# Two cross-attention passes and two MLPs on one core: in each unit of the first MLP the numerator's matmuls move ahead of the next slope's, and GpSimd squares 288 of 960 columns in place of 192

## The chip, the cores and the metric

One core of a Trainium2 chip runs the whole program in one launch. The metric is the device time in microseconds (us); the kernel before takes 2559.63 us (median of 3 runs, 2558.59 to 2561.37). The engines are TensorE (PE in the profile, with its weight loads as PEld), VectorE (DVE), ScalarE (ACT), GpSimd (POOL) and the queue that issues the transfers (SP).

## The reference

`x` is 2 x 12480 tokens of 128 features, `inducing` is 32 x 128. First an attention of the 32 inducing rows over all tokens of a batch (`h = mab(I, x)`), then of all tokens over the 32 rows of `h` (`mab(x, h)`), which gives 24960 x 128 tokens. Two MLPs of width 2048 follow:

```
h = x @ w_in;  h2 = h*h;  h3 = h2*h                     # first MLP
P = a[0] + a[1]*h + a[2]*h2 + a[3]*h3
Q = 1.0 + |b[0]|*|h| + |b[1]|*h2
x = (P / (Q + 1e-6)) @ w_out
h = x @ w_in2;  out = (h * cos(h)) @ w_out2             # second MLP
```

All is float32.

## The kernel before

**Tiling.** Tokens go in 52 groups of 480. A group meets the 2048 hidden features in 8 units; a unit is 2 chunks of 128 features by 480 tokens, that is 128 partitions x 960 columns. So the first MLP has 416 units, and the second as many. Since the token that enters the first MLP is a softmax over 32 rows, `h @ w_in` is folded into small stacked weights (`stack_now`, 96 rows: high part, low part, high part again) that multiply the attention weights (`part_hi`, 96 rows). Three stacks stand there: one gives the hidden value, one the slope (a term linear in h), one the numerator's rest.

**One unit n of the first MLP**, engine by engine:
- TensorE `hidden` (2 matmuls, L1068) writes h into banks 0 and 1, which all units share: it waits until the unit before has been read by `square_ready` and `abs0_ready` (ScalarE) and by `abs1_ready` (VectorE).
- ScalarE `from_hidden`: Square of the first OWN columns of each half (L564; OWN is 384, so 768 of 960 columns), then Abs of the first half (L565, 480 columns). VectorE `absolute` (L790) makes the other 480 columns of |h|; it waits for the Square.
- GpSimd `square_rest` (L409): the other 2 x 96 = 192 columns of the square, from |h|; then `denominator` (L420): square plus |h|, 960 columns.
- ScalarE `log_den` (Ln, L548) and `invert_den` (Exp, L553): one over the denominator.
- TensorE `slope` (2 matmuls) writes into one of two pairs of banks, `num(k)`, taken in turn. It waits for `act_ready` of two units before, that is until the quotient of unit n-2 has been read out of the same banks.
- VectorE `product` (L781) multiplies the slope by the square in place; it waits for `slope_ready` and the square.
- TensorE `numerator` (2 matmuls, L1068 too) adds its stack onto the product; it waits for `prod_ready`.
- VectorE `quotient` (L802) makes the activation; it gives `act_ready`.
- TensorE `end` (2 `matmul` calls that run as 4 passes, L1075) multiplies it by `w_out` into the accumulator; after 8 units ScalarE `keep_y` (L571) reads it out.

**Order.** The order on each engine is written out by hand, one step per k, with units at offsets (HID 5, MAG 4, SLOPE 3, DEN 3, NUM 2, QUO 1). In step k, TensorE does `end(k)`, at most one piece of the next groups' attention (`score2`, L1084, in two steps of 8; `turn_att`, L1092, in two others), `slope(k+3)`, `numerator(k+2)`, `hidden(k+5)`. VectorE does `product(k+2)`, `quotient(k+1)`, `absolute(k+4)`, with small attention operations between (`between`), the largest `keep_att` (L764) behind `absolute`. ScalarE does `log_den(k+2)`, `from_hidden(k+4)`, `invert_den(k+2)`. GpSimd does `square_rest(k+3)`, `denominator(k+3)`, and once per group `part_att` (L425, L427). All are loops over 24 units (3 groups). In 4 of VectorE's rounds (12 groups) it also splits the second MLP's weights (L916, L921) once or twice per group.

The second MLP (L1219 to L1236 and the rest) has its own order and is not touched.

Of the kernel before, what the change touches and what calls it, by code (L numbers as in the profile page):

```python
# [64 lines left out]
TINY_BETA, TINY_SIGMA = 2.0 ** -40, 2.0 ** -46  # L65
SPLIT = GROUP

OWN = 384


HID, MAG, SLOPE, NUM, QUO, DEN = 5, 4, 3, 2, 1, 3
# [18 lines left out]
def group_due(k, at):  # L90
    return (k - at) // GROUP_UNITS if (k - at) % GROUP_UNITS == 0 else None
# [6 lines left out]
def exists_unit(n):  # L98
    return not isinstance(n, int) or 0 <= n < UNITS


def bass_set_attention_two_mlps(nc, x, inducing, w_in, w_out, a, b, w2_in, w2_out, out):
# [3 lines left out]
    with ExitStack() as ctx:  # L106
# [120 lines left out]
        def halves(ap):  # L227
            return ap.rearrange("p (a n) -> p a n", a=2)
# [4 lines left out]
        def num(k):  # L233
            n = 2 + 2 * (k % 2)
            return bank[:, n:n + 2, 0:GROUP]
# [76 lines left out]
        def later(group):  # L312

            return exists(group) and not (isinstance(group, int) and group < 2)
# [78 lines left out]
        def _(pool):  # L393
# [9 lines left out]
            def square_rest(n0, k):  # L403
# [3 lines left out]
                pool.wait_ge(abs1_ready, n + 1)  # L407
                rest = halves(abs_h[k % 3])[:, :, OWN:]
                nc.gpsimd.tensor_tensor(halves(square[k % 3])[:, :, OWN:], rest, rest, ALU.mult).then_inc(square_parted, 1)  # L409

# [100 lines left out]
        def _(act_):  # L511
# [43 lines left out]
            def from_hidden(n0, k):  # L555
# [5 lines left out]
                elif n == 2:  # L561

                    act_.wait_ge(exp_turned, STEPS)
                nc.scalar.activation(halves(square[k % 3])[:, :, 0:OWN], hid[:, :, 0:OWN], ACT.Square).then_inc(square_ready, 1)  # L564
                nc.scalar.activation(abs_h[k % 3][:, 0:SPLIT], bank[:, 0, 0:GROUP], ACT.Abs).then_inc(abs0_ready, 1)  # L565
# [420 lines left out]
        def _(pe):  # L986
# [77 lines left out]
            def from_stack(place_out, i, k, start, stop):  # L1064
                u, place = k % GROUP_UNITS, k // GROUP_UNITS % PLACES
                for t in range(2):
                    w = slice((2 * u + t) * P, (2 * u + t + 1) * P)
                    mm = pe.matmul(place_out[:, t, :], stack_now[:, i, w], part_hi[0:K3, place, :], start=start, stop=stop,  # L1068
                                   skip_group_check=not start)
                return mm  # L1070
# [7 lines left out]
            def score2(g, batch, subs):  # L1078
                if subs[0] == 0:
                    pe.wait_ge(x_fetched, g * 16 + 16)  # L1080
                    if not isinstance(g, int) or g >= 1:
                        pe.wait_ge(att_kept, g)
                for j in subs:
                    mm = pe.matmul(spare[0:SUB, j * M:(j + 1) * M], x_group[:, j * SUB:(j + 1) * SUB], ht[:, batch, :], start=True, stop=True)  # L1084
                if subs[-1] == GROUP_SUBS - 1:
                    mm.then_inc(s2_ready, 1)

            def turn_att(g, subs):
                pe.wait_ge(att_parted, g + 1)
                for j in subs:  # L1090
                    thrice = att[:, j, :, :].rearrange("p r m -> p (r m)")
                    mm = pe.transpose(spare[0:K3, j * SUB:(j + 1) * SUB], thrice, ident[0:SUB, 0:SUB])  # L1092
                if subs[-1] == GROUP_SUBS - 1:
                    mm.then_inc(att_turned, 1)

            def hidden(n0, k):
                n, g = n0 + k, n0 // GROUP_UNITS + k // GROUP_UNITS
                if not isinstance(n, int) or n >= 1:
                    pe.wait_ge(square_ready, n)
                    pe.wait_ge(abs0_ready, n)  # L1100
                    pe.wait_ge(abs1_ready, n)
                else:

                    pe.wait_ge(xt_ready, GROUPS)
                if k % GROUP_UNITS == 0:
                    pe.wait_ge(att_kept, g + 1)
                if isinstance(n, int) and n < GROUP_UNITS:
                    pe.wait_ge(stack_first[PIECES], 2 * PIECES * 16)
                    pe.wait_ge(stack_first[n * 2 * P // PIECE], 16)
                if isinstance(n, int) and 0 <= n - BATCH_GROUPS * GROUP_UNITS < GROUP_UNITS:  # L1110
                    pe.wait_ge(stack_ready[k % GROUP_UNITS], 48)
                from_stack(hid, 0, k, True, True).then_inc(hid_ready, 1)

            def slope(n0, k):
                n = n0 + k
                if not isinstance(n, int) or n >= 2:
                    pe.wait_ge(act_ready, n - 1)
                elif n == 0:

                    pe.wait_ge(exp_ready, STEPS)  # L1120
                else:

                    pe.wait_ge(exp_col_ready, STEPS)
                    pe.wait_ge(h_kept, STEPS)
                from_stack(num(k), 1, k, True, True).then_inc(slope_ready, 1)

            def numerator(n0, k):
                pe.wait_ge(prod_ready, n0 + k + 1)
                from_stack(num(k), 2, k, False, True).then_inc(num_ready, 1)

            def end(n0, k):
                n, g = n0 + k, n0 // GROUP_UNITS + k // GROUP_UNITS
                pe.wait_ge(act_ready, n + 1)
                if k % GROUP_UNITS == 0 and not (isinstance(g, int) and g == 0):
                    pe.wait_ge(y_kept, g)
                product_out(acc, v1, k, act[k % 2]).then_inc(act_used, 1)

            def steps(n0, ks, batch=None):
                for k in ks:
                    if k >= 0:  # L1140
                        end(n0, k)
                    for half in range(2):
                        subs = range(half * GROUP_SUBS // 2, (half + 1) * GROUP_SUBS // 2)
                        g = group_due(k, SCORE + half)
                        if g is not None and later(n0 // GROUP_UNITS + g):
                            group = n0 // GROUP_UNITS + g
                            score2(group, batch if batch is not None else group // BATCH_GROUPS, subs)
                        g = group_due(k, TURN + half)
                        if g is not None and later(n0 // GROUP_UNITS + g):
                            turn_att(n0 // GROUP_UNITS + g, subs)  # L1150
                    if k + SLOPE >= 0 and exists_unit(n0 + (k + SLOPE)):
                        slope(n0, k + SLOPE)
                    if k + NUM >= 0 and exists_unit(n0 + (k + NUM)):
                        numerator(n0, k + NUM)
                    if k + HID >= 0 and exists_unit(n0 + (k + HID)):
                        hidden(n0, k + HID)

# [43 lines left out]
            hidden(0, 3)  # L1201
            fold(1, range(PIECES))
            steps(0, range(-1, 0))
            pe.wait_ge(v1_loaded, 16)
            steps(0, range(0, 1))
            pe.wait_ge(stack_lo, B * STACKS)
            with pe.Fori(0, TURNOVER) as i:
                n0 = pe.snap(i * BODY)
                steps(n0, range(1, BODY + 1), batch=0)
            steps(TURNOVER * BODY, range(1, BODY + 1))  # L1210
            with pe.Fori(TURNOVER + 1, LOOPS) as i:
                n0 = pe.snap(i * BODY)
# [86 lines left out]
            with pe.Fori(0, LOOPS // 2) as i:  # L1299
                n0 = pe.snap(i * 2 * BODY)  # L1300
# [28 lines left out]
```

## Time and profile before

| | |
|---|---|
| median of 3 runs | 2559.63 us |
| the profiled execution's own time | 2556.54 us |
| its span | 2554.7 us |
| TensorE busy / weight loads | 99% / 71% of the span |
| ScalarE | 96% |
| VectorE | 91% |
| GpSimd | 82% |
| granted TensorE clock, mean | 0.999 |
| DMA in the two MLPs | 8 to 17 GB/s in most slices |

Busy time is the time in which at least one operation of the engine is open. Operations of one engine overlap: the next one starts before the end of the one before, so that neither the sum of durations nor a share near 100% tells by itself that an engine has no time left. The first MLP takes about 100 to 1430 us of the span, the second the rest.

### The profile page before, as it was taken

To read this page: it belongs to the slowest core of one execution; us is meant where nothing else is said; L and a number is where in the kernel's file an instruction comes from. 1 tells how busy PE (TensorE), PEld (TensorE's weight loads), DVE (VectorE), ACT (ScalarE), POOL (GpSimd) and SP (SyncE) were. 2 spreads that over 40 slices of the span, in tenths; PEclk is the share of its full clock that TensorE was granted. 3 is DMA by queue.
4 is the path that set the end of the run, shared out by engine and by line. 5 is a ranking of instruction groups with operands and counts; after the bars stand their busy time and mean duration, and the time that the engine had idled before them with its cause. 6 is when DMAs were issued, how large, how long until landed. Compare 5 with 4: busy or idle time off the path is not lost.

```text
span 2554.7 us, 38677 instructions
## 1 busy us (share of the span) xinstructions
PE 2529.0 (99%) x10790; PEld 1812.3 (71%) x10790; DVE 2319.9 (91%) x2712; ACT 2450.9 (96%) x3152; POOL 2101.8 (82%) x1471
## 2 busy tenths in 40 slices
PE   8899999999999999999999999999999999999999
PEld 6566666666666666666665788888888888888887
DVE  5899999999999999999999888888888888888887
ACT  6899999999999999999999999999999999999998
POOL 0588888888888888888888888888888888888886
PEclk9999999999999999999999999999999999999999
DMA  7200000000020000000000000000000000000000
GB/s 223 66 12 8 12 8 12 8 12 8 12 74 16 8 12 8 12 8 12 8 12 1 17 13 12 12 12 12 12 12 12 12 12 12 12 12 12 12 12 16
DMA packets 27816, 48.94 MB, mean 19 GB/s; under 512 B 3352, under 2 KB 12344, under 8 KB 27512
## 3 DMA queue, kind: packets, MB, share of 16 engines
q1 hardware_dynamic: 27768, 48.33, 6.3%
q8 instruction: 26, 0.43, 0.1%
q14 instruction: 22, 0.18, 0.0%
HBM read 18.04 MB, written 12.78 MB: 12 GB/s over the span
## 4 chain that ended last, share of the span: by engine, by line
PE 94%; DVE 3%; issue 2%; DMA 1%; ACT 0%; POOL 0%; SPq 0%; DVEq 0%; POOLq 0%; ACTq 0%
PE bank L1075 24%; PE bank L1068 22%; PE bank L1236 22%; PE bank L1228 21%; PE bank L1084 1%; DVE work L802 1%; PE bank L1219 1%; PE bank L996 1%; PE bank L1092 1%; DMA x_ring<-in_x_dram 1%; PE bank L1025 0%; PE bank L1005 0%; DVE work L790 0%; DVE bank L781 0%; POOL work L420 0%
## 5 line engine op out<-in xcount | busy, mean ns | idle before, releaser
L479 POOL TENSOR_TENSOR act_lo<-work,act_hi 128x960 fp32r<-128x960 f32 (+1 forms) x413 | 831.1, 2013 | 196.7 <-ACT act_hi L647 196.6
L1075 PE MATMUL bank<-work,v 128*128 128x480 f32 x1664 | 737.8, 565 | 0.0
L1068 PE MATMUL bank<-part_hi,stack_now 96*128 96x480 f32 x2496 | 655.4, 397 | 6.5 <-DVE work L802 3.0
L420 POOL TENSOR_TENSOR work<-work 128x960 f32<-128x960 f32 x278 | 621.3, 2235 | 40.7 <-POOL work L409 5.6
L960 DVE SCALAR_TENSOR_TENSOR work<-work,bank 128x960 f32<-128x960 int32 x416 | 479.2, 1152 | 141.5 <-ACT work L634 141.4
L1068 PEld LDWEIGHTS bank<-part_hi,stack_now 96*128 96x128 f32 x2496 | 437.1, 188 | 220.2 <-DVE work L802 167.1
L781 DVE SCALAR_TENSOR_TENSOR bank<-bank,over_c,work 128x960 f32<-128x960 f32 x416 | 509.1, 1224 | 51.1 <-PE bank L1068 45.5
L802 DVE SCALAR_TENSOR_TENSOR work<-bank,coef_a,work 128x960 f32<-128x960 f32 x416 | 501.3, 1205 | 0.2 <-PE bank L1068 0.2
L966 DVE TENSOR_TENSOR work<-work,bank 128x960 f32<-128x960 f32 x416 | 477.5, 1148 | 0.0
L548 ACT ACTIVATE work<-work,made 128x960 f32<-128x960 f32 x416 | 455.7, 1095 | 3.1 <-POOL work L420 2.2
L1075 PEld LDWEIGHTS bank<-work,v 128*128 128x128 f32 x1664 | 313.6, 189 | 202.8 <-issue 178.7
L634 ACT ACTIVATE work<-bank 128x960 int32<-128x960 f32 x416 | 405.1, 974 | 37.2 <-PE bank L1228 37.2
L553 ACT ACTIVATE work<-work 128x960 f32<-128x960 f32 x416 | 419.5, 1008 | 0.1
L638 ACT ACTIVATE work<-work 128x960 f32<-128x960 f32 x416 | 416.2, 1000 | 0.3 <-DVE work L960 0.3
L647 ACT CAST act_hi<-work 128x960 fp32r<-128x960 f32 (+1 forms) x413 | 367.2, 889 | 0.2 <-issue 0.2
L564 ACT ACTIVATE work<-bank 128x768 f32<-128x768 f32 x416 | 334.5, 804 | 16.1 <-PE bank L1068 14.8
L420 POOL TENSOR_TENSOR work<-work,abs_third 128x960 f32<-128x960 f32 x138 | 308.6, 2236 | 20.2 <-POOL work L409 2.9
L1228 PE MATMUL bank<-part_hi,w_hi 128*128 128x480 f32 x832 | 315.1, 379 | 0.7 <-DVE work L966 0.7
L1228 PE MATMUL bank<-part_lo,w_hi 128*128 128x480 f32 x832 | 315.0, 379 | 0.0
L1228 PE MATMUL bank<-part_hi,w_lo 128*128 128x480 f32 x832 | 313.9, 377 | 0.0
L1236 PE MATMUL bank<-act_hi,v_hi 128*128 128x480 f32 x723 | 278.9, 386 | 0.0
L1236 PE MATMUL bank<-act_hi,v_lo 128*128 128x480 f32 x723 | 274.4, 380 | 0.0
(120 smaller groups left out, 2855.7 us busy)
## 6 DMA issues: line engine op xcount, KB each, us to landing
x_group<-tokens_t SPq DMA_DIRECT2D x52, 240.0 KB, 2.2
out_dram<-work SPq DMA_DIRECT2D x52, 240.0 KB, 2.4
x_ring<-in_x_dram SPq DMA_DIRECT2D x28, 240.0 KB, 4.6
work<-in_x_dram SPq DMA_DIRECT2D x24, 240.0 KB, 3.9
w_raw<-in_moe_w_in_dram SPq DMA_DIRECT2D x2, 1024.0 KB, 9.5
stack_now<-first_hi SPq DMA_DIRECT2D x8, 192.0 KB, 3.7
stack_now<-next_hi SPq DMA_DIRECT2D x16, 96.0 KB, 2.2
stack_now<-first_lo SPq DMA_DIRECT2D x4, 192.0 KB, 5.0
```

Source lines behind the costliest of these rows:

```text
L420: nc.gpsimd.tensor_tensor(quot[k % 3], square[k % 3], abs_h[k % 3], ALU.add).then_inc(den_ready, 1)
L479: nc.gpsimd.tensor_tensor(act2_lo[:, k % 2, w], angle[k % ANGLES][:, w], act2_hi[:, k % 2, w].bitcast(F32), ALU.subtract).then_inc(act2_pa ...
L548: nc.scalar.activation(q, q, ACT.Ln, bias=1.0 + EPS_Q, scale=made[:, 5:6]).then_inc(log_ready, 1)
L553: nc.scalar.activation(q, q, ACT.Exp, scale=-1.0).then_inc(inv_ready, 1)
L781: nc.vector.scalar_tensor_tensor(out=num(k), in0=num(k), scalar=over_c2[:, 0:1], in1=halves(square[k % 3]), op0=ALU.add, op1=ALU.mult).the ...
L802: nc.vector.scalar_tensor_tensor(out=halves(act[k % 2]), in0=num(k), scalar=coef_a[:, 0:1], in1=halves(quot[k % 3]), op0=ALU.add, op1=ALU. ...
L960: nc.vector.scalar_tensor_tensor(out=halves(angle[j % ANGLES]), in0=halves(turns[j % 2]), scalar=-2 * pi, in1=buf(j), op0=ALU.mult, op1=AL ...
L966: nc.vector.tensor_tensor(q, q, buf(j), ALU.mult).then_inc(act2_ready, 1)
L1068: mm = pe.matmul(place_out[:, t, :], stack_now[:, i, w], part_hi[0:K3, place, :], start=start, stop=stop, skip_group_check=not start)
L1075: mm = pe.matmul(sums, v[:, 2 * u + t, :], g[:, t * GROUP:(t + 1) * GROUP], start=(2 * u + t == 0), stop=(2 * u + t == CHUNKS - 1))
L1228: mm = pe.matmul(buf(k)[:, t, :], lhs[:, w], rhs, start=(kind == 0), stop=(kind == 2))
L1236: return pe.matmul(sums, lhs[:, c, :], rhs[:, t * GROUP:(t + 1) * GROUP], start=(c == 0 and first), stop=(u == GROUP_UNITS - 1 and last))
```

## The change

OWN goes from 384 to 336: ScalarE squares 2 x 336 = 672 columns of each unit, GpSimd 2 x 144 = 288. And in each step of TensorE's order in the first MLP `numerator(k+2)` stands ahead of `slope(k+3)`; the waits of both stay as they are.

```
-OWN = 384
+OWN = 336
...
+                    if k + NUM >= 0 and exists_unit(n0 + (k + NUM)):
+                        numerator(n0, k + NUM)
                     if k + SLOPE >= 0 and exists_unit(n0 + (k + SLOPE)):
                         slope(n0, k + SLOPE)
-                    if k + NUM >= 0 and exists_unit(n0 + (k + NUM)):
-                        numerator(n0, k + NUM)
                     if k + HID >= 0 and exists_unit(n0 + (k + HID)):
                         hidden(n0, k + HID)
```

## Rows read from the trace of the kernel before

**Rows 1.** Busy time by engine, 300 to 500 us (columns: PE, PEld, DVE, ACT, POOL).
```profile
300.00:500.00 200.00, 199.85 (x723) 124.85 (x722) 192.05 (x236) 197.60 (x266) 175.99 (x140) 1.00 0.03 10
```

**Rows 2.** VectorE in order of time, 705 to 740 us (start, duration, operation).
```profile
705.51 1.21 DVE L802 SCALAR_TENSOR_TENSOR work<-bank,coef_a,work 128x960 f32<-128x960 f32 x1
706.64 0.65 DVE L790 TENSOR_SCALAR abs_third<-bank 128x480 int32<-128x480 int32 x1
707.52 1.23 DVE L781 SCALAR_TENSOR_TENSOR bank<-bank,over_c,work 128x960 f32<-128x960 f32 x1 [0.23 <-PE bank L1068]
708.65 1.21 DVE L802 SCALAR_TENSOR_TENSOR work<-bank,coef_a,work 128x960 f32<-128x960 f32 x1
...
711.79 1.21 DVE L802 SCALAR_TENSOR_TENSOR work<-bank,coef_a,work 128x960 f32<-128x960 f32 x1
...
713.48 0.64 DVE L764 CAST part_hi<-bank 96x480 fp32r<-96x480 f32 x1
714.05 1.21 DVE L781 SCALAR_TENSOR_TENSOR bank<-bank,over_c,work 128x960 f32<-128x960 f32 x1
715.17 1.21 DVE L802 SCALAR_TENSOR_TENSOR work<-bank,coef_a,work 128x960 f32<-128x960 f32 x1
...
718.31 1.21 DVE L802 SCALAR_TENSOR_TENSOR work<-bank,coef_a,work 128x960 f32<-128x960 f32 x1
...
721.66 1.21 DVE L802 SCALAR_TENSOR_TENSOR work<-bank,coef_a,work 128x960 f32<-128x960 f32 x1
...
737.43 1.21 DVE L802 SCALAR_TENSOR_TENSOR work<-bank,coef_a,work 128x960 f32<-128x960 f32 x1
```

**Rows 3.** Matmuls in order of time, 701 to 720 us.
```profile
701.19 0.82 PE L1068 MATMUL bank<-part_hi,stack_now 96*128 96x480 f32 x3
701.84 1.77 PE L1075 MATMUL bank<-work,v 128*128 128x480 f32 x4
...
706.78 1.57 PE L1068 MATMUL bank<-part_hi,stack_now 96*128 96x480 f32 x6
708.19 1.77 PE L1075 MATMUL bank<-work,v 128*128 128x480 f32 x4
709.80 0.37 PE L1092 MATMUL bank<-ident,att 120*96 120x120 f32 x2
...
719.47 0.51 PE L1084 MATMUL bank<-ht,x_group 128*120 128x32 f32 x4
719.81 1.56 PE L1068 MATMUL bank<-part_hi,stack_now 96*128 96x480 f32 x6
```

**Rows 4.** Waits between 300 and 1300 us (total us, times, longest).
```profile
PEld bank L1068 <- DVE work L802: 119.8, 166, 0.8
```

**Rows 5.** Groups of instructions, 300 to 1300 us (busy us, mean ns, idle before).
```profile
L564 ACT ACTIVATE work<-bank 128x768 f32<-128x768 f32 x311 | 249.9, 804 | 9.5 <-PE bank L1068 8.7
...
L565 ACT ACTIVATE work<-bank 128x480 f32<-128x480 f32 x207 | 117.4, 567 | 0.0
...
L409 POOL TENSOR_TENSOR work<-work 128x192 f32<-128x192 f32 x207 | 104.9, 507 | 48.3 <-DVE work L790 48.3
...
L921 DVE TENSOR_TENSOR w_lo<-w_raw,w_hi x13 | 6.4, 493 | 0.0
```

**Rows 6.** GpSimd in order of time, 707 to 711 us.
```profile
707.17 0.39 POOL L425 CAST att<-att_exp 120x256 fp32r<-120x256 f32 x1
...
708.03 0.50 POOL L409 TENSOR_TENSOR work<-abs_third 128x192 f32<-128x192 f32 x1
708.68 2.25 POOL L420 TENSOR_TENSOR work<-work,abs_third 128x960 f32<-128x960 f32 x1
```

**Rows 7.** ScalarE in order of time, 710 to 714 us.
```profile
710.96 1.10 ACT L548 ACTIVATE work<-work,made 128x960 f32<-128x960 f32 x1
711.96 0.79 ACT L564 ACTIVATE work<-bank 128x768 f32<-128x768 f32 x1
...
714.00 1.09 ACT L548 ACTIVATE work<-work,made 128x960 f32<-128x960 f32 x1
```

## The prediction

> **What bounds the kernel now.** I read the busy time of a stretch of the first MLP first, then VectorE, TensorE, GpSimd and ScalarE in order of time, and the waits last.
>
> The busy view ranks TensorE (199.85 of 200 us) and ScalarE (197.60) first [rows 1]. Neither is what closes the period; the reader sees that in the order of time. Take the end of a quotient as zero: 705.51 + 1.21 = 706.72 [rows 2]. The slope's first matmul starts at 706.78, +0.06 [rows 3]: it waited for that quotient, as it does in 166 of some 311 units [rows 4]. The product starts at 707.52, +0.80, and its row says that it waited for the matmul; the next quotient starts at 708.65 and ends at 709.86, +3.14 [rows 2]. That is a closed loop, quotient, slope, product, quotient, of 3.14 us. A plain unit takes just this. In a group of 8 units the quotients stand 3.14 (708.65 to 711.79), 3.38, 3.14, 3.35 apart, and the eight from 711.79 to 737.43 take 25.64 us, 3.205 each [rows 2]. I call the first four units A, B, C, D. B is long because `keep_att` (713.48, 0.64) holds the product back. D is long because `score2` holds the slope back on TensorE.
>
> TensorE alone: 3 matmuls of L1068 take 701.84 - 701.19 = 0.65, 0.217 each. Six behind a wait take 708.19 - 706.78 = 1.41, so the restart (a weight load that nothing hides) costs 1.41 - 1.30 = 0.11. `end` takes 709.80 - 708.19 = 1.61 [rows 3]. TensorE is through at 0.06 + 1.41 + 1.61 = +3.08, the slope may start at 3.14 + 0.06 = +3.20. It is late by nothing, but has only 0.12 us to give in a unit. `turn_att` takes 0.21 (2 of the 0.107 that it issues at), `score2` 0.34 (719.47 to 719.81) and a restart of 0.10 behind it [rows 3]. Check: 3.08 + 0.34 + 0.10 = 3.52 against 3.20 + 0.11 = 3.31 gives 0.21 late, and D is 3.35 - 3.14 = 0.21 longer.
>
> ScalarE alone goes from Ln to Ln in 714.00 - 710.96 = 3.04 [rows 7], less than any unit; GpSimd's pair takes 0.65 + about 2.2 = 2.85 [rows 6].
>
> **The change part by part.** The terms are made against the profiled execution's own 2556.54 us, which lies 3.1 us under the median of the runs.
>
> *ScalarE's shorter Square.* From 480 to 768 columns is 804 - 567 = 237 ns for 288 [rows 5], so 96 columns less are 0.079 us, 33 us over 416 units if ScalarE closed the period. It doesn't: it waits for TensorE ahead of the Square (8.7 us in 1000, L564 [rows 5]) and its own round is 3.04. I take 0 for it, with 33 us as the far end.
>
> The Trainium skill (Perfetto Trace Analysis, section Identifying the Most-Contended Engine) says to take occupancy as the measure for Vector, Scalar and GpSimd, and to work on the highest first. By that rule ScalarE would be the engine to relieve, and the sum would be 2556.5 - 33 = 2523 us in the profiled execution. The trace speaks against it here: a 3.04 us round in a 3.14 us loop looks full only because waiting operations are open.
>
> *Numerator ahead of slope.* Its product ends about 1.1 us before the quotient does, so the two matmuls (0.43) run in front of the slope and are not delayed. What changes is what follows the slope. `hidden` used to start after four matmuls, at 0.06 + 0.11 + 4 x 0.217 = +1.04. Now it is reached at 0.06 + 0.11 + 0.43 = +0.60. But it waits for `absolute`, which VectorE starts behind the same quotient and ends at 706.64 + 0.65 = 707.29, +0.57 [rows 2]. With the 0.06 of a semaphore, and up to 0.05 more since two waits stand in a row, `hidden` starts at +0.63 to +0.68, and pays the restart of 0.11 a second time in the unit. Then hidden 0.43, `end` 1.61, numerator 0.43: TensorE comes to the slope at +3.21 to +3.26. The old order came there at +3.08. The slope may issue at +3.20 and needs its 0.11 of load, which now hides under the numerator's tail, so its limit is +3.31. A plain unit has a margin of 0.05 to 0.10 left and costs nothing. A unit with attention on TensorE has lost its cover:
> - A (turn_att, 0.21): late by 0.21 - 0.075 = 0.14. Before it was 0.
> - B (turn_att again): `keep_att` holds the product to +1.05 in any case: 0.
> - C (score2, 0.34 + 0.10): 0.44 - 0.075 = 0.36 late, less the 0.24 by which B is longer than a plain unit: 0.12. Before 0.
> - D (score2 again): 0.36 less the 0.12 of C: 0.24 late, where it was 0.21: 0.03.
>
> That is 0.29 us per group. In 12 groups VectorE's splitting of weights (0.49 us each [rows 5]) stands in front of A's product and hides A's part: 0.15 there. 40 x 0.29 + 12 x 0.15 = 13.4 us. Bounds: if `hidden` could follow `absolute` without a restart, at +0.63, the slope is reached 0.11 earlier, C loses its term and A keeps 0.03, D 0.02, together 0.05 per group, 3 us; with a load of 0.1 more after the turn and the late end of the wait, A is 0.26 and C 0.14, together 0.43 per group, 19 us.
>
> *GpSimd's longer square.* 192 columns take 0.507 [rows 5]; 768 more of the denominator take 2.25 - 0.51 = 1.74, 2.26 ns per column, so 96 more are 0.22 us (estimate; strictly in proportion 0.25). Its round goes from 2.85 to 3.07, under 3.14, so it isn't the bound in plain units. But once per group `part_att` stands between, 708.03 - 707.17 = 0.86 [rows 6], and there GpSimd is late already: the denominator ends at 708.68 + 2.25 = 710.93 and Ln starts at 710.96, on its heels [rows 6, 7]. Two squares lie ahead of that point without slack between, so Ln comes 0.41 later (0.22 + 0.19 after a little slack), at 711.37. The Square follows 1.00 later [rows 7], at 712.37, ends 0.72 later at 713.09, and `absolute` can start at 713.15. Without this it would start 0.08 before the end of A's quotient, at 709.86 + 3.28 - 0.08 = 713.06. So it is 0.09 late; `keep_att` and B's product behind it too, and nothing hides that. 40 x 0.09 = 3.6 us; in the 12 groups A is long enough. Bounds: 0 if the square costs under 0.17 more, and with the old, short A (3.14) it would be 0.23 x 40 = 9 us. GpSimd then catches up 0.07 to 0.3 per unit before its next `part_att`.
>
> Next late is nothing new on VectorE: Exp ends some 0.7 us before the quotient wants it. The second MLP stays as it is.
>
> Sum: 2556.5 + 13.4 + 3.6 = 2573.5 in a profiled execution, and with the 3.1 us to the median 2576.6, say 2577 us.
>
> **The rivals.**
> 1. ScalarE is the bound after all, and the time falls: 2559.6 - 33 = 2526 us. For it: 197.6 of 200 us busy. The place is Square in each unit, the price 0.079 us, and it decides if the quotient waits for Exp, or `absolute` for the Square, in plain units. Against it: the rows of VectorE show a wait for TensorE only. A milder form, TensorE's gap of 0.7 us on the weight loads being filled with useful work and D's 0.21 us given back, would be worth at most 52 x 0.21 = 11 us, 2549. It needs `hidden` not to wait for `absolute`. Chance of both together 0.07.
> 2. No change: the semaphore and the load at `hidden` overlap better than I hold, and GpSimd's lag stays under the slack: 0 to 5 us, 2560 to 2564. For it: margins of 0.1 us decide everything here. Chance 0.14.
> 3. The wait at `hidden` costs 0.1 us more than taken (a restart that includes the semaphore's second instruction). Then the margin of plain units is gone and each pays 0.03 to 0.05, 12 to 20 us more: 2589 to 2597. For it: none of the rows shows `hidden` behind such a wait. Against it: the wait of the slope shows 0.06 + 0.11 in all. Chance 0.12.
>
> **How the numbers follow.** My forecast, slower by 8 to 26 us, has the chance 0.67; its own range is 2568 to 2586. The range to hold 8 in 10 takes in most of "no change" and the nearer part of rival 3: 2560 to 2590. 0.2% is about what a measurement can tell here, 5.1 us. Faster by more than that 0.07, within it 0.14, slower by more 0.79.
>
> **What would show it.** Behind the change, in the order of time of a plain unit: two matmuls of L1068 ahead of the quotient's end, two behind it, then a gap on the weight loads of L1068 that `absolute` (L790) ends, and 3.14 us from quotient to quotient as before. A at 3.28, B at 3.4 to 3.5, C at 3.26, D at 3.38. In the waits, PEld of L1068 for L790 is new, and of 0.1 us or so. L564 falls to about 725 ns and L409 rises to about 725 ns. `absolute` of A waits for L564. The span of the second MLP stays. I am wrong if plain units shorten below 3.14 (then VectorE's loop wasn't closed by the slope), if `hidden` shows no wait for L790, or if all units grow alike (rival 3).

## The result and the profile after

The changed kernel takes 2587.64 us (median of 4 runs, 2581.70 to 2588.11) against 2559.11 for the kernel before: 1.011 of its time, 95% interval 1.0098 to 1.0123, or 28.5 us more. 2577 was forecast, with 2590 as the upper end. The profiled execution took 2581.70, its span is 2579.9. It is the quickest of the four and lies 25.2 us over the profiled execution before (2556.54), so its trace has 25 us to explain, not 28.5.

The loss is all in the first MLP. The last quotient ends at 1451.3 us of the span in place of 1425.9; from there to the end it is 1128.6 us, before 1128.8.

Busy time of the same stretch as in [rows 1], columns as there:

```profile
300.00:500.00 200.00, 199.54 (x710) 117.74 (x709) 187.86 (x230) 190.22 (x261) 183.25 (x140) 1.00 0.03 10
```

ScalarE has 7.4 us less, GpSimd 7.3 us more, and neither helped. TensorE's matmuls still look full. Its weight loads fell from 722 to 709 in number, 2%, which is the loss itself; the time in which they are open (second figure) fell by more, 124.85 to 117.74, since two loads behind a wait overlap (0.30 us for the pair in the rows below, 0.19 for one alone) and a unit has two waits now. The granted clock is unchanged.

VectorE in order of time, one group (compare [rows 2]):

```profile
719.15 1.21 DVE L802 SCALAR_TENSOR_TENSOR work<-bank,coef_a,work 128x960 f32<-128x960 f32 x1
720.27 0.65 DVE L790 TENSOR_SCALAR work<-bank 128x480 int32<-128x480 int32 x1
721.33 1.23 DVE L781 SCALAR_TENSOR_TENSOR bank<-bank,over_c,work 128x960 f32<-128x960 f32 x1 [0.41 <-PE bank L1068]
722.47 1.21 DVE L802 SCALAR_TENSOR_TENSOR work<-bank,coef_a,work 128x960 f32<-128x960 f32 x1
...
725.85 1.20 DVE L802 SCALAR_TENSOR_TENSOR work<-bank,coef_a,work 128x960 f32<-128x960 f32 x1
...
729.13 1.21 DVE L802 SCALAR_TENSOR_TENSOR work<-bank,coef_a,work 128x960 f32<-128x960 f32 x1
...
732.52 1.21 DVE L802 SCALAR_TENSOR_TENSOR work<-bank,coef_a,work 128x960 f32<-128x960 f32 x1
...
735.64 1.21 DVE L802 SCALAR_TENSOR_TENSOR work<-bank,coef_a,work 128x960 f32<-128x960 f32 x1
...
738.96 1.19 DVE L802 SCALAR_TENSOR_TENSOR work<-bank,coef_a,work 128x960 f32<-128x960 f32 x1
...
742.09 1.21 DVE L802 SCALAR_TENSOR_TENSOR work<-bank,coef_a,work 128x960 f32<-128x960 f32 x1
...
745.22 1.21 DVE L802 SCALAR_TENSOR_TENSOR work<-bank,coef_a,work 128x960 f32<-128x960 f32 x1
```

The quotients stand 3.32 (A), 3.38 (B), 3.28 (C), 3.39 (D), 3.12, 3.32, 3.13 and 3.13 apart. Plain units keep their 3.14; the sixth, 3.20 before, has grown too. The product of A waits 0.41 for TensorE, where a plain one waits 0.23.

TensorE's weight loads in order of time, around a quotient that ended at 717.21 (0.05 ahead of the third row):

```profile
716.50 0.19 PEld L1068 LDWEIGHTS bank<-part_hi,stack_now 96*128 96x128 f32 x1 [0.21 <-issue]
716.91 0.19 PEld L1068 LDWEIGHTS bank<-part_hi,stack_now 96*128 96x128 f32 x1 [0.21 <-issue]
717.26 0.30 PEld L1068 LDWEIGHTS bank<-part_hi,stack_now 96*128 96x128 f32 x2 [0.17 <-DVE work L802]
717.89 0.30 PEld L1068 LDWEIGHTS bank<-part_hi,stack_now 96*128 96x128 f32 x2 [0.33 <-issue]
```

The numerator's two loads, the slope's two behind the quotient, a gap of 0.33 us, hidden's two. The gap is the new wait: hidden's first load starts 0.115 us behind the end of `absolute` (median over 256 units). It carries the name "issue" and not that of L790, since the wait for `absolute` sits on a separate semaphore instruction ahead of the load, of 51 ns, which starts 0.04 behind `absolute`:

```profile
L1101 PEldq EVENT_SEMAPHORE  x409: 51/51/51, 100.4 to 1441.3; - x137
```

Over 1000 us of the stretch:

```profile
PEld bank L1068 <- issue: 124.0, 490, 0.6
DVE bank L781 <- PE bank L1068: 45.4, 144, 0.5
...
PEld bank L1068 <- DVE work L802: 36.7, 122, 0.6
...
ACT work L548 <- POOL work L420: 27.4, 86, 0.4
```

The 119.8 us of waiting for the quotient [rows 4] fell to 36.7, and 124.0 us under "issue" are new. Not all of that is the wait at `hidden`: sorted by the load that they precede, 67 us (224 gaps) stand ahead of hidden's first load, and 57 us (266 gaps, 0.21 each) ahead of the numerator's two, which now follow `end` and are loaded at the pace of its passes. The last line is Ln waiting for the denominator; ScalarE, relieved, waits for GpSimd. The changed operations themselves (columns as in [rows 5]):

```profile
L564 ACT ACTIVATE work<-bank 128x672 f32<-128x672 f32 x305 | 217.2, 712 | 0.0
...
L409 POOL TENSOR_TENSOR work<-work 128x288 f32<-128x288 f32 x204 | 136.4, 668 | 27.3 <-DVE work L790 24.7
```

The Square is 0.09 shorter, GpSimd's square 0.16 longer (0.22 was estimated).

One table serves all that follows. It gives the mean distance between the ends of neighbouring quotients in us, worked out from each trace's L802 records, over 32 early groups, and for the 12 late ones, in which VectorE also splits weights, unit A and the whole group.

```
                      A     B     C     D     5th   6th   7th   8th   group   late A  late group
before                3.14  3.37  3.14  3.35  3.14  3.20  3.14  3.14  25.62   3.51    25.99
after                 3.32  3.39  3.33  3.37  3.14  3.29  3.14  3.14  26.12   3.85    26.62
e1 order only         3.33  3.37  3.33  3.37  3.14  3.30  3.14  3.14  26.11   3.52    26.29
e2 OWN only           3.14  3.54  3.14  3.35  3.14  3.20  3.14  3.14  25.78   3.84    26.32
e3 after, short abs   3.14  3.15  3.36  3.35  3.14  3.20  3.14  3.14  25.64   3.59    26.07
e4 before, short abs  3.14  3.26  3.23  3.35  3.14  3.21  3.14  3.14  25.60   3.27    25.72
e5 wait written first 3.26  3.43  3.25  3.37  3.14  3.20  3.14  3.14  25.93   3.84    26.46
e6 att wait moved     3.33  3.39  3.34  3.37  3.14  3.21  3.14  3.14  26.05   3.85    26.55
e7 small split        3.32  3.39  3.34  3.37  3.14  3.29  3.14  3.14  26.13   3.78    26.56
e8 split moved        3.14  3.37  3.14  3.34  3.14  3.20  3.14  3.14  25.61   3.14    25.61
```

### The profile page after: what moved, and what is told of

Read it like the earlier page. It is cut to its first block, busy times and chain, and to the rows that moved or that the text cites. A ratio compares the mean times of both kernels' runs of the same rounds, so it can differ in the third digit from the quotient of the medians.

```text
span 2579.9 us, 38677 instructions
## 1 busy us (share of the span) xinstructions
PE 2553.8 (99%) x10790; PEld 1780.7 (69%) x10790; DVE 2323.4 (90%) x2712; ACT 2428.3 (94%) x3152; POOL 2172.7 (84%) x1471
## 4 chain that ended last, share of the span: by engine, by line
PE 94%; DVE 3%; issue 2%; POOL 1%; ACT 0%; DMA 0%; DVEq 0%; SPq 0%; POOLq 0%; ACTq 0%
PE bank L1075 24%; PE bank L1068 23%; PE bank L1236 22%; PE bank L1228 21%; PE bank L1084 1%; DVE work L802 1%; PE bank L1219 1%; PE bank L996 1%; DVE bank L781 1%; PE bank L1092 1%; POOL work L420 1%; PE bank L1025 0%; PE bank L1005 0%; DVE work L790 0%; DMA x_ring<-in_x_dram 0%
## 5 line engine op out<-in xcount | busy, mean ns | idle before, releaser
L1068 PE MATMUL bank<-part_hi,stack_now 96*128 96x480 f32 x2496 | 784.5, 435 | 7.9 <-DVE work L802 3.0
L1068 PEld LDWEIGHTS bank<-part_hi,stack_now 96*128 96x128 f32 x2496 | 413.2, 189 | 267.0 <-issue 173.5
L802 DVE SCALAR_TENSOR_TENSOR work<-bank,coef_a,work 128x960 f32<-128x960 f32 x416 | 500.8, 1204 | 0.0
L564 ACT ACTIVATE work<-bank 128x672 f32<-128x672 f32 x416 | 296.4, 712 | 5.0 <-PE bank L1068 4.9
```

Of the source, the lines that this page charges most:

```text
L802: nc.vector.scalar_tensor_tensor(out=halves(act[k % 2]), in0=num(k), scalar=coef_a[:, 0:1], in1=halves(quot[k % 3]), op0=ALU.add, op1=ALU. ...
```

## The experiments

The theory: the new order makes `hidden` wait for `absolute` and TensorE restart twice per unit; that uses up TensorE's slack, and units with more on TensorE run late. GpSimd's longer square adds a lag behind `part_att`. The main rivals: the loss is GpSimd's alone, or it comes from elsewhere in the order.

### One part alone: e1 and e2

```
 e1: the changed kernel with            e2: the kernel before with
-OWN = 336                             -OWN = 384
+OWN = 384                             +OWN = 336
```

> Only the order of numerator and slope is changed, OWN stays at 384. Theory: the order takes hidden's cover, so units A, B's neighbour C and the unit behind the att_kept wait grow as in the changed kernel (A 3.32, C 3.32, D 3.37, and 3.28 for the sixth of a group), GpSimd does not lag (Ln of A at its old place), and the late groups' A stays near 3.52: 20 to 24 us over before. Rival (the loss is the longer GpSimd square): within 3 us of before. Rival (both parts pay alike, without common cover): 14 us, half of the 28.

> Only OWN goes to 336, the order is the old one. Theory: the denominator behind part_att ends 0.4 us later, absolute of unit A waits for the Square, keep_att and B's product come 0.2 us later in 40 groups, and in the 12 late groups VectorE's split of the weights waits 0.3 us longer for GpSimd: 10 to 14 us over before, so that the two parts alone sum to more than both together (each hides some of the other). Rival (ScalarE bounds, the shorter Square pays): 10 to 30 us under before. Rival (GpSimd has room): within 3 us.

e1: 2582.94 us, ratio 1.0090 (1.0076 to 1.0104), 24 us over the 2558.84 of the kernel before, run beside it. e2: 2566.66 us, ratio 1.0037 (1.0026 to 1.0047), 8 us over. So the order is the larger part, and the shorter Square pays nothing. 24 + 8 = 32 is more than the 28.5 of both, but these medians hardly tell 32 from 28.5; the table does. Early groups grow by 0.49 in e1 and 0.16 in e2, and by 0.50, not 0.65, with both: there the two share cover. In late groups they add up (0.30 + 0.33 = 0.63). e1 has A, C, D and the sixth unit of the changed kernel, and late A as before. e2 has a longer B (3.54) and late A (3.84), and nothing else. e2's loss was expected at 10 to 14 us and is 8 by the medians. Its eight runs lie in two bunches, five at 2566 to 2567 and three at 2571. The profiled one is of the upper bunch, and there the stretch from the first quotient to the last is 10.1 us longer than before, as the table has it (40 x 0.16 + 12 x 0.33 = 10.4).

Why B in e2: ScalarE, then GpSimd, then VectorE of e2 in order of time.

```profile
305.99 1.09 ACT L548 ACTIVATE work<-work,made 128x960 f32<-128x960 f32 x1 [0.37 <-POOL work L420]
306.99 0.71 ACT L564 ACTIVATE work<-bank 128x672 f32<-128x672 f32 x1
```

```profile
303.70 2.25 POOL L420 TENSOR_TENSOR work<-work 128x960 f32<-128x960 f32 x1
```

```profile
306.46 1.21 DVE L802 SCALAR_TENSOR_TENSOR work<-bank,coef_a,work 128x960 f32<-128x960 f32 x1
307.73 0.66 DVE L790 TENSOR_SCALAR abs_third<-bank 128x480 int32<-128x480 int32 x1
308.31 0.64 DVE L764 CAST part_hi<-bank 96x480 fp32r<-96x480 f32 x1
308.87 1.21 DVE L781 SCALAR_TENSOR_TENSOR bank<-bank,over_c,work 128x960 f32<-128x960 f32 x1
```

The denominator ends at 305.95, Ln starts at 305.99, the Square ends at 307.70 and `absolute` starts at 307.73, where it would have started at 307.59 (0.08 ahead of the quotient's end, as at 706.64 in [rows 2]). `keep_att` and the product follow it. This is the prediction's second term, here with the short A: 0.14 in these rows, 0.17 in the mean of B. In the changed kernel A is 0.19 longer and hides it: B is 3.39, 0.02 over before. Its Square in A,

```profile
722.82 0.71 ACT L564 ACTIVATE work<-bank 128x672 f32<-128x672 f32 x1
```

ends at 723.53, and `absolute` starts at 723.59, 0.09 ahead of the quotient's end (722.47 + 1.21 = 723.68), which is where it starts without any wait. So the sign that the prediction named for this term shows in e2 and not in the changed kernel.

### The wait at hidden: e3 and its control e4

```
-  abs_h[k % 3][:, SPLIT:],               bank[:, 1, 0:GROUP]
+  abs_h[k % 3][:, SPLIT:SPLIT+GROUP//2], bank[:, 1, 0:GROUP//2]     (VectorE's absolute)
```

The 240 columns left out are written once, with a constant, at the kernel's start; so part of the denominator is not the reference's.

> The changed kernel, with VectorE's part of |h| cut from 480 to 240 columns; the other 240 are left out (they hold a constant). It ends 0.25 us earlier, so hidden no longer waits for it. Theory: the wait ahead of hidden and its second restart are gone, A is 3.14 to 3.17 and the sixth unit 3.20; what is left is GpSimd's lag: 8 to 12 us over the next kernel. Rival (the loss comes from somewhere else in the new order, not from hidden's wait): 24 to 28 us over the next kernel, as the changed kernel is over the one before.

> The control for the last one: the kernel before with the same 240 columns left out. Theory: plain units stay at 3.14 since the loop quotient, slope, product doesn't hold absolute; B is 0.17 shorter, and C gets that back as a delay on TensorE: 0 to 3 us under before. Rival (VectorE's busy time bounds): 416 x 0.25 = 104 us under before.

e3: 2559.68 us, ratio to before 1.0003 (0.9994 to 1.0012). e4: 2554.74 us, 0.9980 (0.9971 to 0.9989). The new order and OWN cost 4.9 us once `absolute` ends before `hidden` needs it, and 28.5 us when it doesn't. A and the sixth unit are back at their old length, and B and C together (6.51 as before; 6.72 in the changed kernel). The waits of the stretch from 300 to 1300 us in e3 (L1070 is L1068 there) have 41.4 us under "issue":

```profile
PEld bank L1070 <- issue: 41.4, 199, 0.3
```

Of these, 33 us stand ahead of the numerator's second load, and 8 us ahead of hidden's first, where the changed kernel has 67. D is still 3.35 in e3, and its early groups are no shorter than those of e4: even with hidden's wait nearly gone the new order gives nothing back.

One thing e3 does not keep apart: GpSimd's square waits for `absolute` too, so a shorter `absolute` also takes GpSimd's lag away. That the order pays at `hidden` rests on e3 together with e1, where GpSimd's part is the old one, and with e5 below, where only a wait moves.

In e4, `absolute` is 0.25 shorter in each of 416 units, and the gain is 4 us, not 104: its busy time bounds nothing. e3's distance to e4, 4.9 us, is 3 under what was expected, and e4's gain is 1 over. In e4 late A fell by 0.24 (2.8 us in 12 groups), which was not foreseen: GpSimd starts its square sooner there, and the denominator for which the split waits (below) ends 0.87 us behind the quotient in place of 1.10. In e3 the early groups carry no lag any more (25.64 against 25.60); the late ones carry it all, 12 x 0.35 = 4.2 us.

### The semaphore instruction: e5 and e6

```
 e5, in hidden:                         e6: the att_kept wait of hidden
+  pe.wait_ge(abs1_ready, n)               is issued in end() of the same step
   pe.wait_ge(square_ready, n)          +  if (k + HID) % GROUP_UNITS == 0:
   pe.wait_ge(abs0_ready, n)            +      pe.wait_ge(att_kept, ...)
-  pe.wait_ge(abs1_ready, n)
```

> The changed kernel, with the wait for VectorE's |h| written first at hidden, so that it should sit on the weight load itself and not on the separate semaphore instruction ahead of it, which takes 0.076 us after it is released. Theory (hidden's wait for absolute is what the new order pays): hidden's load issues at +0.61 in place of +0.68, TensorE reaches the slope 0.07 earlier, and A, C and the sixth unit are 0.05 to 0.07 shorter each: 7 to 11 us under the changed kernel, near 2578 us. Rival (the order of two satisfied waits is worth nothing, or the gap is weight loading): within 2 us of the changed kernel.

> The changed kernel, with the wait for the copied attention (att_kept) taken from hidden to the end of the same step, 2 us earlier, where it costs nothing. Theory: the sixth unit of each group is 3.28 because hidden ahead of it has two semaphore instructions behind each other (+0.78 in place of +0.68); with one it is 3.20 as before: 4 us under the changed kernel, all in this unit. Rival (the sixth unit is long for VectorE's sum and reciprocal): no change.

e5: 2578.01 us, ratio to before 1.0068 (1.0054 to 1.0082), 9.6 us under the changed kernel. e6: 2583.48, 1.0093 (1.0078 to 1.0109), 4.2 under. Both are what the wait at `hidden` predicts. e6's interval overlaps that of the changed kernel (1.0098 to 1.0123), so its gain rests on the table, where the sixth unit alone changes by more than 0.01 (3.29 to 3.21, 52 x 0.08 = 4.2). The weight loads of e5:

```profile
714.38 0.30 PEld L1068 LDWEIGHTS bank<-part_hi,stack_now 96*128 96x128 f32 x2 [0.29 <-DVE work L802]
714.95 0.30 PEld L1068 LDWEIGHTS bank<-part_hi,stack_now 96*128 96x128 f32 x2 [0.27 <-DVE work L790]
```

and its `absolute`:

```profile
714.25 0.65 DVE L790 TENSOR_SCALAR work<-bank 128x480 int32<-128x480 int32 x1
```

The first wait written sits on the load itself. The load issues at 714.95, 0.05 behind 714.25 + 0.65, and the wait has L790's name now. In the changed kernel a quotient ends at 719.15 + 1.21 = 720.36 and `absolute` at 720.92; hidden's pair of loads starts there, by this row, at 721.04, 0.12 behind it:

```profile
721.04 0.30 PEld L1068 LDWEIGHTS bank<-part_hi,stack_now 96*128 96x128 f32 x2
```

By the medians it is 0.115 in the changed kernel (but ahead of the sixth unit) and 0.053 in e5: the wait's place costs 0.06. It is worth 0.06 in A and 0.08 in C. B grows by 0.04 in e5, as the prediction's second term would have it with a shorter A. In the waits between 300 and 1300 us, hidden's part has a name now and the rest of "issue" is the numerator's:

```profile
PEld bank L1068 <- issue: 57.1, 268, 0.2
...
PEld bank L1068 <- DVE work L790: 36.4, 152, 0.3
...
PEld bank L1068 <- DVE abs_third L790: 15.9, 63, 0.3
```

The sixth unit falls by 0.09 in e5 and is explained by e6: ahead of it `hidden` waits for `att_kept` too, on a second semaphore instruction, and its load starts 0.22 behind `absolute` in the changed kernel. With that wait moved away it starts at 0.12 and the unit is 3.21.

### The split of the weights: e7 and e8

```
 e7 (on the changed kernel): of the pieces that VectorE splits, those ahead of A's
     product have half the columns, those ahead of C's one and a half times as many
 e8 (on the kernel before):
-  if k % GROUP_UNITS == 1 or k % GROUP_UNITS == GROUP_UNITS - 1:   # C and A, 6 pieces a round
+  if k % GROUP_UNITS == 1:                                         # C alone, 3 pieces of double size
```

> The changed kernel, where the split of the second MLP's weights that stands ahead of A's product in the 12 late groups has half its columns (the others go to the split ahead of C's product). Theory (VectorE waits until GpSimd's denominator has ended): the operation still ends when the denominator does, its record is 0.9 to 1.0 us in place of 1.09, late A 3.70 to 3.78 in place of 3.83, 1 us in all. Rival (the operation itself is slow): its record halves to 0.55, late A falls to 3.35, 5 to 6 us.

> The kernel before, with all of this splitting ahead of C's product, where GpSimd waits for |h| and holds nothing, in pieces of twice the size. Theory (GpSimd's denominator is what VectorE's split waits for): late A falls from 3.49 to 3.14, C grows by 0.05 to 0.2 for the larger piece: 2 to 4 us under the kernel before, so faster than both. Rival (the operation costs what it costs wherever it stands): within 1 us of before.

e7: 2587.85 us, ratio to before 1.0110 (1.0094 to 1.0125), the same as the changed kernel. That is what was expected, within what the times can tell (1 us less). The three pairs below are VectorE's split ahead of A's product and GpSimd's denominator beside it, in the kernel before, the changed one and e7:

```profile
1147.38 0.75 DVE L921 TENSOR_TENSOR w_lo<-w_raw,w_hi  x1
```

```profile
1145.73 2.25 POOL L420 TENSOR_TENSOR work<-work 128x960 f32<-128x960 f32 x1
```

```profile
1113.79 1.09 DVE L921 TENSOR_TENSOR w_lo<-w_raw,w_hi  x1
```

```profile
1112.48 2.25 POOL L420 TENSOR_TENSOR work<-work,abs_third 128x960 f32<-128x960 f32 x1
```

```profile
1119.21 1.02 DVE L921 TENSOR_TENSOR w_lo<-w_raw,w_hi  x1
```

```profile
1117.88 2.26 POOL L420 TENSOR_TENSOR work<-work,abs_third 128x960 f32<-128x960 f32 x1
```

The split ends 0.15, 0.15 and 0.09 behind the denominator (1148.13 and 1147.98; 1114.88 and 1114.73; 1120.23 and 1120.14), whenever it began and, in e7, with half the columns. It does so in all 12 late groups of each kernel; in four of them the split is the copy L916, with 0.83 us before and 1.17 in the changed kernel. Ahead of C's product, where GpSimd waits for |h|, the same operation takes 0.28:

```profile
1128.27 0.28 DVE L921 TENSOR_TENSOR w_lo<-w_raw,w_hi  x1
```

So it doesn't work for 1.09 us, it stands for 0.94 of them (1113.79 to 1114.73). Late A follows the denominator in every variant that splits there with whole pieces: it is 2.40 or 2.41 more than the time from the quotient to the denominator's end (1.10 before, 1.45 in the changed kernel, 0.87 in e4, 1.18 in e3). The Trainium skill (SBUF — State Buffer, section SBUF: two separate sides) gives a reason: VectorE and GpSimd share a pair of SBUF ports as an exclusive lock. Whichever starts first, a GpSimd operation that reads SBUF or a VectorE operation with two SBUF inputs or in a two-port mode, holds the pair for its whole instruction, and the other is blocked. The trace agrees for the case in which GpSimd started first, at both sizes of the piece; no row here shows the other.

e8: 2555.42 us, ratio to before 0.9980 (0.9971 to 0.9989): 4.7 us under the kernel before (2 to 4 were expected), so quicker than both. Late A is 3.14, and late C, which I feared would grow by 0.05 to 0.2, is 3.15. Its split, at double the size:

```profile
1131.93 0.41 DVE L921 TENSOR_TENSOR w_lo<-w_raw,w_hi  x1
1132.27 1.22 DVE L781 SCALAR_TENSOR_TENSOR bank<-bank,over_c,work 128x960 f32<-128x960 f32 x1
```

## Why the prediction was right, and where it was short

**What bounds the kernel** held. The loop quotient, slope, product stays at 3.14 in every variant, with ScalarE relieved (e2) or VectorE relieved (e4). ScalarE's shorter Square is worth nothing; rival 1 fell. Its milder form, a filled gap that gives D's 0.21 back, fell with e3: hidden's wait is nearly gone there and D is 3.35. Rival 2, no change, fell with the measured time. The margin of Exp, which the prediction put at some 0.7 us ahead of the quotient, is 0.94 at least; nothing hung on it.

**Numerator ahead of slope** held as a mechanism, and its size was short: 11.6 + 1.8 us forecast, 24 measured (e1). The prediction said that it would be wrong if `hidden` showed no wait for L790. By that name it shows none; the wait is there, under "issue", and e5 brings the name out. Three terms:
- *The margin of a plain unit* was put at 0.05 to 0.10 and reckoned at 0.075. It was about 0.02, if A's delay is turn_att's 0.21 less the margin (estimate: 0.21 - 0.19). The semaphore instruction ahead of hidden's load costs 0.06 where I took 0 to 0.05 and reckoned with the middle; that is most of the 0.05 that is missing. A is late by 0.19 and not 0.14, C by 0.19 and not 0.12. D at 0.02 fits 0.03. Plain units themselves did not grow, so rival 3 (each pays) fell, though its cause, the second instruction, is what made A and C dearer.
- *The sixth unit* was costed at nothing. The wait for `att_kept` in `hidden` was not counted as an instruction of TensorE's queue: 0.09 x 52 = 4.7 us, 4.2 by e6.
- *The late groups' A* I called hidden behind the split. It is, for the order: 3.52 in e1.

**GpSimd's longer square** was given 3.6 us, all in B. Alone it costs 8 to 10 (e2), 6.4 of them in the early groups, where the prediction's bound for the short A was 9. Beside the new order it costs B next to nothing (3.39 for 3.37 in e1): A is 0.19 longer where 0.14 was taken, and the square 0.16 longer where 0.22 was taken, and the prediction itself gave 0 for less than 0.17. The price comes where I had put 0: VectorE's split waits for the later denominator, 0.34 x 12 = 4.1 us. I took the 0.49 mean of L921 in [rows 5] as its cost; it was a mean of 0.28 and 0.75, and two such durations for one operation were the sign of a wait inside the record. I had also named "A is long enough" as the reason for no cost there: true of `absolute`, not of what stands behind it.

**The sum**: A 0.19, B 0.02, C 0.19, D 0.02 and the sixth 0.09 make 0.50 per early group (26.12 - 25.62), x 40 = 20 us; late 26.62 - 25.99 = 0.63, x 12 = 7.6. That is 27.6, and from the first quotient to the last the traces differ by 27.5. Their spans differ by 25.2 only, since the changed kernel's first quotient ended 2.2 us earlier (89.8 for 92.0 us). That the forecast of 2577 lies as near as 10.6 us owes something to chance: GpSimd's 3.6 us stood in the wrong place and came to 4.1 in another.

**Open**: C is about 3.30, 3.30, 3.40 in turn over three groups in the changed kernel, and TensorE's loop round is three groups long. In its trace the loop's branch back (0.21 us) stands in B of a group 13 times, and the C behind it is the long one all 13 times (3.36 to 3.44). Behind the two branches that leave a loop C is 3.29. In the kernel before the branches stand in the same place and C stays 3.14. So a cost of the branch that was hidden before fits; no run tested it. Nor is it settled why the profiled execution is 6 us under the other three. In the ten traces the first quotient ends at 89.8 to 97.2 us, earliest in the changed kernel, while the part behind the last quotient differs by 0.4 us; the other three have no trace.

## What to carry to other kernels

An order that lets an engine work while it waits pays only if the work behind it isn't waiting for something later: here the numerator went into a gap of some 0.2 us of TensorE (+3.08 to +3.31 in the prediction), and `hidden` moved ahead of the end of `absolute`, which had always come early enough. Before reordering, write down for each instruction behind the moved one how early its last input was; count each further wait as an instruction, and write first the wait that is released last, so that it sits on the operation itself. Where one form of an operation has two durations, look at what the other engine holds in the long ones before taking the mean.

## What the hardware showed that was not expected

- Of several waits on a TensorE operation, the one written first sat on the weight load (0.053 us from `absolute` to the load, e5), the others on a semaphore instruction ahead of it (0.115; 0.22 with two such instructions). The profile puts the time behind such an instruction under "issue", together with gaps that are no wait for another engine.
- VectorE's split of the weights stands still until GpSimd's running operation ends, and its record is open all the while: 0.28 us free, 0.75 and 1.09 beside a denominator that ends later.
- GpSimd's square takes 668 ns for 288 columns and 507 for 192: 1.7 ns per column, less than the 2.26 of the denominator that the estimate used.
